# Moving half of the h copies to ScalarE, a third staging buffer, and another order on VectorE

## The reference, cut to what matters

```python
for t in range(S):                                   # S = 768, 4 batches x 8 heads, head size 48
    cur = einsum('bhd,bhe->bhde', u * kt, vt)
    y[:, :, t] = einsum('bhd,bhde->bhe', rt, state + cur)
    state = wt[..., None] * state + einsum('bhd,bhe->bhde', kt, vt)

h = x @ w_in                                         # 384 -> 2048
g = h * tanh(log1p(exp(h)))
x2 = g @ w_out                                       # 2048 -> 384

logits = x2 @ w_gate                                 # 8 experts, 384 tokens each, greedily by size of logit
for e in range(8):
    out[mask_e] = maximum(x2[mask_e] @ w1[e], 0) @ w2[e]   # 384 -> 1024 -> 384
```

## Time and profile before

| what | value |
|---|---|
| median of three runs | 844.1 us (843.27 to 844.26) |
| the profiled execution's own time | 845.52 us |
| its span, first to last instruction | 843.8 us |
| mean granted TensorE clock | 0.975 |
| TensorE busy | 787.3 us (93%) |
| VectorE busy | 649.3 us (77%) |
| ScalarE busy | 403.4 us (48%) |

### The profile page before, as it was taken

How to read it: one execution, slowest core, us unless ns; L and a number is a source line. 1 busy time by engine, 2 the same in 40 slices (tenths; PEclk the granted TensorE clock), 3 DMA queues, 4 the chain that set the end, 5 groups by cost and what they waited for, 6 DMA issues and landing times.

```text
span 843.8 us, 16959 instructions
## 1 busy us (share of the span) xinstructions
PE 787.3 (93%) x6744; PEld 577.0 (68%) x6744; DVE 649.3 (77%) x1123; ACT 403.4 (48%) x655; POOL 284.9 (34%) x244
## 2 busy tenths in 40 slices
PE   8799999999998999999899999996799999999995
PEld 7788877777877686877677677753465665666662
DVE  8979988888979797969798897757777777766220
ACT  2457647575665757574747576920111211212221
POOL 3315362624444343344262536001212313213311
PEclk9999999999999999999999999998699999999999
DMA  9952246363554636281838262303324244235510
GB/s 311 335 197 61 73 142 246 107 212 142 179 196 139 235 98 266 76 299 58 317 101 298 86 233 91 132 20 149 138 91 179 79 156 181 98 135 206 193 41 29
DMA packets 47790, 133.48 MB, mean 158 GB/s; under 512 B 5344, under 2 KB 19808, under 8 KB 45664
## 3 DMA queue, kind: packets, MB, share of 16 engines
q1 hardware_dynamic: 38880, 93.07, 31.3%
q0 software_dynamic: 5376, 34.61, 11.1%
q10 hardware_dynamic: 3456, 4.72, 1.5%
HBM read 97.78 MB, written 34.60 MB: 157 GB/s over the span
## 4 chain that ended last, share of the span: by engine, by line
PE 35%; DVE 31%; issue 13%; ACT 12%; DMA 6%; POOL 1%; SPq 1%; DVEq 0%; ACTq 0%; POOLq 0%
PE bank L414 34%; DVE inv L925 7%; ACT t_sb L733 6%; DMA stage<-in_moe_w 5%; DVE cum L916 4%; DVE h_sb L995 3%; DVE t_sb L1002 3%; DVE stage L1023 2%; DVE kdiv L933 2%; DVE att L948 2%; ACT g_hi L733 2%; ACT L814 1%; PE bank L664 1%; DVE rdec L940 1%; ACT L822 1%
## 5 line engine op out<-in xcount | busy, mean ns | idle before, releaser
L414 PE MATMUL bank<-x_hi,win_hi 128*128 128x256 f16 x576 | 159.3, 277 | 11.6 <-DVE h_sb L995 7.6
L414 PE MATMUL bank<-x_lo,win_hi 128*128 128x256 f16 x576 | 159.0, 276 | 0.0
L414 PE MATMUL bank<-x_hi,win_lo 128*128 128x256 f16 x576 | 158.9, 276 | 0.0
L1446 POOL TENSOR_TENSOR g_lo<-t_sb,g_hi 128x512 f16<-128x512 f32 x88 | 119.8, 1384 | 87.8 <-ACT g_hi L733 87.8
L414 PE MATMUL bank<-wout_hi,g_hi 128*128 128x392 f16 (+1 forms) x416 | 129.8, 319 | 0.8 <-issue 0.8
L414 PE MATMUL bank<-wout_lo,g_hi 128*128 128x392 f16 (+1 forms) x416 | 129.6, 318 | 0.0
L414 PE MATMUL bank<-wout_hi,g_lo 128*128 128x392 f16 (+1 forms) x416 | 129.6, 319 | 0.0
L1430 POOL TENSOR_TENSOR dv<-v_tok,dot 128x384 f32<-128x384 f32 x24 | 39.6, 1649 | 203.0 <-DVE dot L955 203.0
L733 ACT ACTIVATE g_lo<-bank 128x384 f16<-128x384 f32 x64 | 31.4, 490 | 144.1 <-PE bank L414 144.1
L733 ACT ACTIVATE g_hi<-t_sb 128x512 f16<-128x512 f32 x96 | 56.0, 623 | 90.4 <-DVE t_sb L1002 86.8
L1002 DVE TENSOR_TENSOR t_sb<-t_sb,h_sb 128x512 f32<-128x512 f32 x96 | 93.4, 1001 | 6.3 <-ACT t_sb L733 4.2
(11 more groups left out here) (179 smaller groups left out, 1467.1 us busy)
## 6 DMA issues: line engine op xcount, KB each, us to landing
stage<-in_moe_w SPq DMA_DIRECT2D x32, 768.0 KB, 7.3
w_split<-stage SPq DMA_DIRECT2D x32, 768.0 KB, 5.4
wt<-in_w_turned SPq DMA_DIRECT2D x24, 258.0 KB, 6.5
kt<-in_k_turned SPq DMA_DIRECT2D x24, 256.0 KB, 6.2
rt<-in_r_turned SPq DMA_DIRECT2D x24, 256.0 KB, 6.4
r_tok<-in_r SPq DMA_DIRECT2D x24, 192.0 KB, 7.5
k_tok<-in_k SPq DMA_DIRECT2D x24, 192.0 KB, 8.5
v_tok<-in_v SPq DMA_DIRECT2D x24, 192.0 KB, 5.1
```

What stands on the lines that cost most here:

```text
L414: return nc.tensor.matmul(*a, **k)
L1446: G.tensor_tensor(g_lo[:, j * GW:(j + 1) * GW], t_sb[:, j * GW:(j + 1) * GW], g_hi[:, j * GW:(j + 1) * GW], ALU.subtract).then_inc(s["glo" ...
```

## The change

1. **Copies.** `copied` on VectorE leaves out odd tiles; ScalarE gets a `copied` of its own for them (semaphore `hca`), ahead of `arctan` and `tanh` of its place. The new helper `copy_of` waits for the right semaphore; TensorE's `tile`, ScalarE's `tanh` and VectorE's `gated` use it.
2. **Pieces.** Three staging buffers each way instead of two; the third pair is the idle `fold_w`. A piece is read as soon as the buffer of the third before it is free. VectorE makes remainders at places 5, 6, 8 (and 14), one or more places later than before; in round 11 ScalarE works at 1, 3, 5, 7 and VectorE at 2, 4, 6, 8. Rounds 2 to 9 have three pieces, rounds 10 and 11 four. SyncE issues the loads of `w`, `k`, `r` of a chunk ahead of the first piece, and splits the two loads by token round the second.
3. **Order.** On VectorE `dots(n0)` moves from place 5 to 4, `sum_x(n0)` to 6 and `new_state(n0)` to 7, and the eight `gated` stand together, two at each of the places 9 to 12, with `sum_x(n1)` and `new_state(n1)` between them; `low_x(n1)` and `products` come behind them. On ScalarE `turn_x(n0)` moves from place 8 to 7.

TensorE's instructions and their order stay as they are.

```diff
+RING = 3
+        def copy_of(eng, i, j):
+            eng.wait_ge(s["hca" if j % 2 else "hcp"], NJ // 2 * i + j // 2 + 1)
-            begin = [3 * (k - 2) + max(0, k - 8) for k in (i, i + 1)]
-            return range(begin[0], min(begin[1], PIECES))
+            begin = [3 * (k - 2) + max(0, k - 10) for k in (i, i + 1)]
+            return range(begin[0], begin[1])
-        SPLIT_SLOTS = (1, 3, 5, 12)
+        def split_slots(i):
+            return ((1, 3, 5, 7), (2, 4, 6, 8)) if i == NI - 1 else ((1, 3, 5, 12), (5, 6, 8, 14))
-            return stage[n % 2][:, :]
+            return (stage[0], stage[1], fold_w[0])[n % RING][:, :]
...
             for i in range(NI - 2):
+                turned(2 * i + 5)
                 pieces_of(i, slice(0, 1))
-                turned(2 * i + 5)
+                rows_rk(2 * i + 4)
                 pieces_of(i, slice(1, 2))
-                by_token(2 * i + 4)
+                rows_v(2 * i + 4)
                 pieces_of(i, slice(2, 3))
                 by_token(2 * i + 5)
...
+            def copied(i, j):                                   # ScalarE
+                if j % 2 == 0:
+                    return
+                act.wait_ge(s["h"], NJ * i + j + 1)
+                if i >= 1:
+                    act.wait_ge(s["g"], NJ * (i - 1) + j + 1)
+                A(h_sb[:, j * GW:(j + 1) * GW], hb[HB[j]][:, :], scale=0.5).then_inc(s["hca"], 1)
...
                 if slot < NJ:                                   # ScalarE, turn
-                    tanh(i, slot)
+                    copied(i, slot)
                     if slot >= 1:
                         arctan(i, slot - 1)
+                    tanh(i, slot)
...
             def copied(i, j):                                   # VectorE
+                if j % 2:
+                    return
```

More of the change, by code:

```diff
@@ L203, in moe_chain @@
         wst = [sem(f"s_wst{i}") for i in range(4)]
-        praw = [sem(f"s_praw{i}") for i in range(2)]
-        pout = [sem(f"s_pout{i}") for i in range(2)]
+        praw = [sem(f"s_praw{i}") for i in range(RING)]
+        pout = [sem(f"s_pout{i}") for i in range(RING)]
         w1g = [sem(f"s_w1g{i}") for i in range(2)]
@@ L834, in turn @@
                       ).then_inc(s["foldhi"], 1)
[L835 to L842, removed]
+                for n in split_now(i, slot, 0):
+                    act.wait_ge(praw[n % RING], 16 * (n // RING + 1))
+                    if n >= RING:
+                        act.wait_ge(pout[n % RING], 16 * (n // RING))
+                    elif n == 2:
+                        act.wait_ge(s["fold"], 4)
+                    else:
+                        act.wait_ge(s["woutlo"], 3 + n)
+                    A(split_out(n)[:, 0, :], split_raw(n), scale=(SW1, SW2)[n // 2 % 2]).then_inc(s["phi"], 1)
             def finish(i, step):
@@ L1017, in expert_piece @@
             def expert_piece(i, slot):
-                if slot - 2 not in SPLIT_SLOTS:
-                    return
-                for n in split_now(i, slot - 2):
+                for n in split_now(i, slot, 1):
                     dve.wait_ge(s["phi"], n + 1)
@@ L1083, in turn @@
                         elif slot == 4:
+                            dots(n0)
                             query_side(n1)
[L1085 to L1090 removed]
+                        elif slot == 6:
+                            sum_x(n0)
+                        elif slot == 7:
+                            new_state(n0)
+                    if slot in (3, 5, 7) and i == 1:
+                        split_piece(4 + (slot - 3) // 2)
+                    expert_piece(i, slot)
                     return
+                if slot == 8:
+                    expert_piece(i, slot)
                 if 1 <= i < NI - 1:
@@ L1118, in turn @@
                     gated(i, 3)
-                elif slot == 11 and 1 <= i < NI - 1:
-                    sum_x(n1)
-                    new_state(n1)
-                elif slot >= 12:
-                    if slot == 12 and 1 <= i < NI - 1:
+                elif slot == 11:
+                    gated(i, 4)
+                    if 1 <= i < NI - 1:
+                        sum_x(n1)
+                    gated(i, 5)
+                    if 1 <= i < NI - 1:
+                        new_state(n1)
+                elif slot == 12:
+                    gated(i, 6)
+                    gated(i, 7)
+                    if 1 <= i < NI - 1:
                         low_x(n1)
-                    gated(i, slot - 8)
+                        if with_next:
+                            products(n2)
+                elif slot >= 13:
                     if i == NI - 1 and slot == SLOTS - 1:
@@ L1504, in _ @@
             G.partition_all_reduce(gmax[:, :], amax[:, :], P, RMAX).then_inc(s["maxout"], 1)
-            for i in range(2):
-                pool.wait_ge(pout[i], 16 * (PIECES // 2))
+            for i in range(RING):
+                pool.wait_ge(pout[i], 16 * len(range(i, PIECES, RING)))
             def weights(p):
```

59 lines of the change are left out of this document (25 added, 34 removed).

## The result

The changed kernel takes 815.5 us (median of four runs, 812.96 to 815.78) against 844.2 of the kernel before on the same chip: a ratio of 0.9651, 95% interval 0.9626 to 0.9676. That is 28.7 us saved where I forecast 23, and the time lies just under my range of 816 to 836. The profiled execution has a span of 814.0 us against 843.8, 29.8 less, and this is the sum to be explained.

What follows compares the result with a forecast made beforehand. TensorE's work was taken as the floor, only its waiting winnable: 25.9 - 2 (masks) - 0.5 (last round) - 0.5 (unseen waits) = 22.9 us, so 844.1 becomes 821 us (chance 0.70); range 816 to 836, own range 817 to 826.

Steps and rivals of the forecast that it cites:

- What bounds the kernel: TensorE's work is the floor at 93% busy; only its waiting can be won, at most 25.9 us in the rounds.
- The restart of a wait: TensorE's 26 waits in rounds 2 to 10: each costs 0.12 us beyond its idle time, 3.1 us in all.
- The masks of n1: VectorE's masks at place 9, up to 0.82 us of wait: half the remainder kept, 2 us stay, ends 0 and 4.
- The reserves: Held back from the saving: 0.5 us for the last round (0 to 2), 0.5 for a wait or two not seen.
- The second part: Program after round 11: same instructions, 0 us, with 1 us either way for how the clock falls at its start.
- The first copy of a round: VectorE's copy of tile 0: `gated` moved ahead of `low_x(n1)` brings it up to 5 us earlier; 6.1 us of waits go.
- `ktok`: ScalarE's copy that TensorE awaits for 7.9 us: over 3.1 us earlier, all nine waits and the start-up's go.
- ScalarE's wait for the read: ScalarE's piece at place 5 waits 3.40 us; a third buffer removes this (30.6 us in all), `x_hi(n0)` 2 to 3 earlier.
- Copies on ScalarE's path: Bank of tile 3 wanted for tile 6: ScalarE needs 5.1 us of 8, so cost 0 with 3 us of room.
- Partial: Rival: only VectorE's relief at the round's start works; `ktok` and masks wait as before; 837 us, chance 0.12.
- ScalarE holds the bank: Slower rival: a piece's read issued late delays copy 3, about 3.5 us a round at tile 6; 872 us, chance 0.05.
- The port: Rival: VectorE's run of products and GpSimd's remainders lock each other out, perhaps 1 us a round; 830 us, chance 0.08.

Runs made afterwards that it cites:

- delay run: Changed kernel plus two needless 128x768 products on VectorE ahead of the second chunk's masks, rounds 1 to 10: 817.7 us.
- ring alone: Kernel before with three staging buffers and SyncE's new order, VectorE's remainders and the fourth pieces as before: ratio 0.9867.
- places alone: Kernel before with two buffers, VectorE's remainders moved to places 5, 6, 8 and fourth pieces only in rounds 10 and 11: ratio 1.0297.

## Why the prediction was nearly right, and where it was not

**What bounds the kernel: right.** TensorE's waits in rounds 2 to 10 and what follows from them are 27.8 of the 29.8 us. Rounds 4, 7 and 10 take 41.29 us (forecast 41.4), rounds 3, 6 and 9 42.65 (43).

**Where the number failed: sizes, all on one side.** The step that failed is the sum "20.5 + 3.1 + 1.6 + 0.75 = 25.9 us, is the most that the rounds can give": without its 0.75 for the start-up it allows 25.2 us in rounds 2 to 10, and they gave 27.8. On top of it I kept back 3.0 us, and none of it was spent. My sum was 22.9 and the median gave 28.7; against the profiled execution (29.8 of span) the terms are:

- *The restart of a wait*: taken as 0.12 "for the short waits", though the only row that I had, 1.53 lost for 1.37 idle, says 0.16. The delay run shows 0.16 at a wait of 0.26 us too, and 0.05 behind it. Laid over the changed kernel's trace, start for start, the 26 waits of the kernel before lose 5.4 us beyond their idle time, 0.17 to 0.23 each, in place of 3.1: 2.3 missed. This is the largest, and it was a choice against my own row. With it the waits, their restarts and the slow stretch make 20.5 + 5.4 + 1.6 = 27.5 against 27.8 measured; the 0.3 is what rounds 2 and 3 are late by (0.12 and 0.18) ahead of their first wait in the list.
- *The masks of n1*: I kept 2.0 us; none is left. I had `x_hi(n0)` 2 to 3 us earlier; it came 4.1 earlier (22.73 against 26.87), since the wait for the read and the time ahead of `ktok` were both gained.
- *The reserves*: 0.5 for waits not seen and 0.5 for round 11; neither was spent. Round 11 is as long as before, to 0.01 us. ScalarE waits for no read of a piece in the rounds, round 11 included.
- *The second part*: 0.9 shorter, taken as 0 with 1 us either way. Ahead of round 2, 1.0 instead of 0.75, but not by the reason given: the start-up's `ktok` wait grew from 0.75 to 1.2. Both are no larger than what executions of one kernel differ by. A second profiled execution of the changed kernel has no such `ktok` wait and begins round 2 at 114.34, 0.77 us sooner; the kernel without the new order takes 286.6 us from `amax` on in one profiled execution and 285.5 in another. So these 1.9 us can't be put down to the change.

2.3 + 2.0 + 0.5 + 0.5 + 0.9 + 0.25 = 6.45, of 29.8 - 22.9 = 6.9; 0.3 of the rest is 27.8 against 27.5, and rounding makes up what is left. My own range ended at "the ceiling of 25.9"; a ceiling that is a sum of rows with an assumed price is no ceiling.

**The first copy of a round: right in its outcome, wrong in its reason.** I had the run of `gated` bring it up to 5 us earlier. It is about 1 earlier (4.06 us into the round against 5.0). From `low_x(n1)` to it VectorE needs 8.25 us instead of 11.8, but `low_x(n1)` itself stands at 38.46 us instead of 38.05, behind the four products, and the round is 2.2 us shorter. The runs put it in its place: the kernel without the new order is at the floor too, and the ring alone takes these waits from 6.1 to 1.6 us, because ScalarE's `x_hi(n1)` comes 1.9 us earlier. Either lever does. The forecast needed neither to be named rightly, as the wait was at most 1.8: that the term of 6.1 us came true was luck as far as its reason goes.

**`ktok`: right.** The remainder of place 3 was in front of it: the ring alone leaves 7.3 us of waits, places alone or on top of the ring leave none in rounds 2 to 10, the copies alone leave 2.0. It comes 3.07 us earlier in the changed kernel (15.55 against 18.62); "over 3.1" was the forecast.

**ScalarE's wait for the read: right that it goes, and undersold.** I used it for the masks of n1 alone. It is the root of two kinds of waits: with the ring alone, 12.6 of the 27.8 us go. That the copies alone would clear the waits for tile 0, as I expected before that run, was wrong: 6.6 us are left.

**Copies on ScalarE's path: right, cost 0.** But they bring nothing in rounds 2 to 10 either once pieces and order are there; what they buy is round 11, 1.4 us with the order (37.0 against 35.6) and, with a part of it the clock's, 2.4 without (38.0).

**The rivals.** *Partial* (ScalarE as late as before) fell: it is 3 to 4 us earlier. *ScalarE holds the bank* fell: with all eight copies on it there is no wait. Its mechanism, a read issued too late, is real and was met elsewhere, with places and two buffers: there it costs 3%. *The port* is there in the trace and hidden: products that took from 0.92 to 1.63 us take 1.55 each at the end of the run, and `kdiv` and `rdec` 1.41 and 1.48 us (`kdiv` 0.69 at 292.69, where GpSimd does nothing). The Trainium skill ("SBUF — State Buffer", on the port pair that VectorE and GpSimd share) has it that the one stands still while the other works, and those durations beside GpSimd's remainders agree in kind. Agreement ends there: GpSimd, partly beside these products, takes 6.75 us for five remainders, 1.35 each, and 1.16 for one without them (at 324.28): it is slowed too, and by less. TensorE has no wait from it.

**The parts do not add.** As ratios times 844.2 us they give singly 4.6 (copies), 17.8 (pieces) and 18.3 us (order), 40.7 together, and all three give 28.7 to 29.5. Any two give 26.3 to 31.1. The excess that a round can lose is bounded by the floor, and each part takes away some of the same waits. The copies show the other side: alone they shorten some waits and lengthen the next.

What stays open: the order in the changed kernel is of no use that a run could show; the versions without it and with all copies on ScalarE are as fast, none faster. What SyncE's order does by itself, apart from the third buffer, no run shows. Why the clock falls behind one wait and not behind another of the same length stays open as well.

## What to carry to other kernels

When the bound engine's waits are short and many, look for the one wait further back that makes several of them late: here a read into a ring of two buffers, 3.4 us on ScalarE, which cost TensorE waits at two other places. Move the release of a buffer later only together with a deeper ring; alone, the same edit that helps by 7 us beside a third buffer costs 25, most of it because TensorE's clock falls behind the longer waits. And price a wait by the distance of the two starts around it against the same pair without a wait, for every wait alike.

## What the runs showed of the hardware

- A wait of TensorE costs 0.16 us more than its recorded idle time and a little at the next operation, at an idle time of 0.26 as at 0.58 to 1.37 (round 6 before and after: 0.44 + 0.06 lost for 0.28, 0.75 + 0.04 for 0.58, 0.88 + 0.06 for 0.72; round 9, at tile 3: 1.54 + 0.01 for 1.37).
- Waits of 1.0 to 2.0 us were followed in some places, not in all, by a stretch at the lower clock, though TensorE was busy in it: 1.6 to 1.7 us lost each (kernel before, round 2; order alone, rounds 5 and 9). Waits of 1.7 to 4.7 us, with places alone, were followed by it or ended in it in 8 of 9 cases. Without waits the share is 1.00 in every round.
- ScalarE copies 128x512 float32 from a bank in 0.589 us (mean of 48) and VectorE in 0.665 (mean of 96 before); the Trainium skill ("ScalarE: Activation LUTs", Rules for kernel authors) would have such a product on VectorE, and here it is faster where it now stands.
